# Attention with fp32 products: probabilities and values weighed without splitting, the first 28 units' scores from keys and queries as loaded

## The chip, the cores and the metric

One NeuronCore of a Trainium2 chip. The time is the device time of one execution in microseconds (us); less is better. The kernel of before was timed in three executions and profiled in a further one.

## What is computed

Attention with a window and sinks, then two feed-forward layers, all in fp32 (shapes: 2 batches, 8 heads, 768 positions, 64 wide; 4 sinks, window 128; 1536 tokens, model 512 wide, hidden 2048).

```python
scores = (1/8) * q @ k.T                      # per batch and head
keep = (key < n_sink) | (0 <= query - key < window)
a = softmax(where(keep, scores, -1e9)); attn = a @ v
x = relu(attn @ w_in)**2 @ w_out              # layer 1
h = x @ w2_in                                 # layer 2
g = (a0 + a1 h + a2 h^2 + a3 h^3) / (1 + |b0||h| + |b1|h^2)
out = g @ w2_out
```

## The kernel before

TensorE's fast type here, fp32r, holds only the high bits of an fp32 number. So every operand is split into a high part (written as fp32r) and a low part (the number minus the high part), and a product is three matmuls: high by high, high by low, low by high (`PASSES`). For the scores the key sits in rows 0 to 63 as high part and in rows 64 to 127 as low part, and the query stands twice, so two matmuls do (`bq_hi`, `bq_lo`, line 1169).

Attention is cut into 96 units `u`, each one head of one tile of 128 queries; 8 heads make a tile, 6 tiles a batch; i = (u // 8) % 6 is the tile's place in its batch. A unit looks at up to 288 keys: 32 sink columns, the 128 keys before, the 128 of its own place. Tiles with i = 0 look at 128 keys, with i = 1 at 256, the others at 288. Four units make a group `k`; keys, queries and values arrive by group. A unit goes through this chain, where slot `s` starts unit s and works on earlier ones:

- PE `score` (L1170), DVE `scores` (L920: scale, mask, minimum per row; it writes `bprobs`, in which a unit's columns are 4 elements apart), ACT `exp` (L649, in place)
- PE `turn_p` two slots later (L1185, and L1187 for the sinks of four units at once), ACT `pT_part` (L642: high part), DVE `pT_part` (L929: low part)
- PE `weigh` three slots later: for each tile of 128 keys three matmuls of 64 columns (L1202); each fourth unit with i of 2 or more adds three of 256 columns for the sinks (L1212). In all 176 key tiles and 16 sink products.
- per tile of queries: DVE `finish`, then `tile_out` (four transposes, a high part, a low part) into `xT`.

The first 28 units (`LEAD`) run alone, slot after slot. The other 68 are laid between the matmuls of layer 1 (`first1` L1125, `second1` L1137), at places given by `events` and `slot_of`, in blocks 0 to 2 of four. Layer 2 follows and touches no attention.

The splitting is done by several engines. POOL splits each group's keys and queries (`split_kq`: L439, L441, L443, L452), its values (`split_v`: L461, L464) and the sinks; for the first three groups ACT and DVE split the queries (`early_q`: L625, L828). The 16 weight tiles of layer 1 are split by ACT (high, L634) and POOL (low, L426), the low parts of the first two by DVE during the lead (L858). All DMAs are issued by SP in one order written out by hand (`banded`); `load_kq` and `load_v` wait until the split of two groups before has freed the buffer. Every engine enters `banded` through a branch on `path_ready`, which DVE sets at line 823.

## Time and profile before

| | us |
|---|---|
| median of three executions | 725.2 (723.95 to 727.53) |
| profiled execution | 728.82 |
| its span, first to last instruction | 726.8 |
| PE busy | 695.8 (96%) |
| DVE busy | 487.5 (67%) |
| ACT busy | 413.5 (57%) |
| POOL busy | 372.4 (51%) |

The profiled execution lies 2.0 us above its span and 3.6 us above the median. A timeline gives the start of an instruction, its time and its engine; several alike in a row are merged (x6), so the start of the next row tells how long they took in truth. A matmul's own time is modelled and includes the way through the array; for its price the distance of the starts is read. Most of the span falls to four stretches: the lead up to 67, blocks 0 to 2 of layer 1 with the other units up to 375, block 3 without units up to 443, then layer 2.

### The profile page before, as it was taken

Reading aid. Unit: us, or ns where it says so; the run is one execution under the profiler, and the core shown is the slowest. Engines: PE = TensorE matmul, PEld = TensorE weight load, DVE = VectorE, ACT = ScalarE, POOL = GpSimd, SP = SyncE. Lnnn points to the kernel's source line nnn. Section 1 sums busy time; section 2 is a strip of 40 time slices with the busy share of each in tenths; the row PEclk is TensorE's granted clock in tenths of the full one; section 3 lists DMA queues with packets and bytes.
Section 4 is the critical chain, followed back from the end, with each engine's and each line's share of the span. In section 5 each row is a group of like instructions: output and inputs, shape, how many; then the busy total and the mean of one; then the engine's idle time right before and its main releaser. Section 6 shows DMA issues by size and latency. Waiting matters only on the chain.

```text
span 726.8 us, 10617 instructions
## 1 busy us (share of the span) xinstructions
PE 695.8 (96%) x3888; PEld 662.6 (91%) x3888; DVE 487.5 (67%) x714; ACT 413.5 (57%) x861; POOL 372.4 (51%) x376
## 2 busy tenths in 40 slices
PE   3999989999999999999999997999999999999996
PEld 2998989999999999999999997889988998998995
DVE  6664465564465554554445665799989889898985
ACT  3764446554545544554432223677787787778774
POOL 5666157675242350530002221777867767776773
PEclk9999999999999999999999998999999999999999
DMA  6654211112221113100003332000210120001001
GB/s 204 212 216 158 86 37 37 44 37 73 88 88 37 37 37 124 37 8 1 1 1 130 131 116 92 1 1 1 88 43 1 45 86 1 1 1 43 1 1 44
DMA packets 14507, 43.50 MB, mean 60 GB/s; under 512 B 1648, under 2 KB 4976, under 8 KB 13936
## 3 DMA queue, kind: packets, MB, share of 16 engines
q1 hardware_dynamic: 14448, 42.74, 16.9%
q8 instruction: 34, 0.56, 0.3%
q14 instruction: 25, 0.20, 0.1%
HBM read 36.44 MB, written 6.29 MB: 59 GB/s over the span
## 4 chain that ended last, share of the span: by engine, by line
PE 84%; DVE 6%; POOL 4%; issue 3%; ACT 2%; DMA 1%; POOLq 0%; DVEq 0%; SPq 0%; ACTq 0%
PE h_ps L1125 22%; PE y_ps L1137 17%; PE y_ps L1356 16%; PE s_ps L1125 8%; PE o_ps L1202 6%; PE o_ps L1125 4%; PE s_ps L1170 3%; PE s_ps L1185 3%; PE y_ps L1202 1%; DVE s_ps L874 1%; DVE sq L837 1%; PE o_ps L1212 1%; PE y_ps L1170 1%; POOL weights L426 1%; DVE o_ps L874 1%
## 5 line engine op out<-in xcount | busy, mean ns | idle before, releaser
L1125 PE MATMUL h_ps<-xT,weights 128*128 128x384 f32 x960 | 194.8, 346 | 3.4 <-DVE xT L961 1.5
L1125 PEld LDWEIGHTS h_ps<-xT,weights 128*128 128x128 f32 x960 | 171.5, 192 | 6.2 <-issue 3.0
L1137 PE MATMUL y_ps<-hid,weights 128*128 128x384 f32 x768 | 156.3, 343 | 0.0
L1356 PE MATMUL y_ps<-weights,hid 128*128 128x512 f32 x576 | 144.7, 395 | 4.1 <-POOL hid L553 4.1
L1137 PEld LDWEIGHTS y_ps<-hid,weights 128*128 128x128 f32 x768 | 134.9, 190 | 0.0
L1356 PEld LDWEIGHTS y_ps<-weights,hid 128*128 128x128 f32 x576 | 107.1, 188 | 26.1 <-POOL hid L553 5.9
L649 ACT ACTIVATE bprobs<-bprobs,neg_max 128x288 f32<-128x288 f32 (+2 forms) x96 | 73.5, 766 | 58.4 <-DVE neg_max L920 56.9
L837 DVE TENSOR_TENSOR sq<-sq 128x384 f32<-128x384 f32 x64 | 44.6, 696 | 80.2 <-ACT sq L581 80.1
L439 POOL TENSOR_SCALAR bq_hi<-kq_raw 128x512 fp32r<-128x512 f32 x21 | 13.4, 640 | 148.0 <-PE s_ps L1170 132.2
L544 POOL TENSOR_TENSOR q_buf<-h_abs,q_buf 128x384 f32<-128x384 f32 x64 | 65.0, 1016 | 45.3 <-ACT q_buf L604 43.5
L553 POOL TENSOR_TENSOR hid<-p_buf,hid 128x384 fp32r<-128x384 f32 x64 | 65.6, 1025 | 41.2 <-ACT hid L760 40.8
L874 DVE RECIPROCAL s_ps<-q_buf 128x384 f32<-128x384 f32 x32 | 82.0, 2561 | 3.3
L843 DVE TENSOR_TENSOR hid<-sq,hid 128x384 fp32r<-128x384 f32 x64 | 55.8, 872 | 37.8 <-ACT hid L586 37.8
L581 ACT ACTIVATE sq<-h_ps 128x384 f32<-128x384 f32 x64 | 31.4, 491 | 79.8 <-PE h_ps L1125 79.7
L920 DVE CUSTOM_DVE_ANT_0 bprobs<-s_ps,band_bias 128x288 f32<-128x288 f32 (+2 forms) x82 | 51.2, 624 | 36.3 <-PE s_ps L1170 36.2
L1125 PE MATMUL s_ps<-xT,weights 128*128 128x384 f32 x384 | 73.7, 341 | 0.0
L1125 PEld LDWEIGHTS s_ps<-xT,weights 128*128 128x128 f32 x384 | 69.7, 191 | 2.6
L1202 PE MATMUL o_ps<-bv,bpT 128*128 128x64 f32 x456 | 70.5, 293 | 0.2 <-DVE o_sb L944 0.2
L548 POOL TENSOR_TENSOR p_buf<-p_buf,h_sb 128x384 f32<-128x384 f32 x64 | 65.0, 1016 | 0.0
L1202 PEld LDWEIGHTS o_ps<-bv,bpT 128*128 128x128 f32 x456 | 64.7, 212 | 0.3 <-issue 0.3
L421 POOL TENSOR_SCALAR weights<-weights_raw 128x1024 fp32r<-128x1024 f32 x16 | 16.8, 1052 | 90.0 <-DMA weights_raw<-in_w_pack 90.0
L586 ACT ACTIVATE hid<-sq 128x384 fp32r<-128x384 f32 x64 | 33.5, 524 | 48.8 <-DVE sq L837 48.8
(104 smaller groups left out, 1082.2 us busy)
## 6 DMA issues: line engine op xcount, KB each, us to landing
weights_raw<-in_w_pack SPq DMA_DIRECT2D x32, 512.0 KB, 3.7
kq_raw<-in_kq_pack SPq DMA_DIRECT2D x24, 512.0 KB, 3.9
bv_raw<-in_v_pack SPq DMA_DIRECT2D x24, 128.0 KB, 2.1
y_scratch<-xT SPq DMA_DIRECT2D x2, 1536.0 KB, 5.3
xT<-y_scratch SPq DMA_DIRECT2D x2, 1536.0 KB, 6.6
out_y<-out_stage SPq DMA_DIRECT2D x3, 768.0 KB, 3.5
out_y<-out_stage SPq DMA_DIRECT2D x3, 256.0 KB, 2.0
sink_raw<-in_vs_pack SPq DMA_DIRECT2D x2, 256.0 KB, 5.1
```

The costliest lines, as they stand in the source:

```text
L544: pool.tensor_tensor(q_buf[:, i % RING, :], h_abs[:, i % RING, :], q_buf[:, i % RING, :], ALU.mult).then_inc(qmul_ready, 1)
L548: pool.tensor_tensor(p_buf[:, i % RING, :], p_buf[:, i % RING, :], h_sb[:, i % RING, :], ALU.mult).then_inc(pmul_ready, 1)
L553: pool.tensor_tensor(hid2[:, i % RING, LO, :], p_buf[:, i % RING, :], hid2[:, i % RING, HI, :].bitcast(F32), ALU.subtract).then_inc(hid_re ...
L649: nc.scalar.activation(at, at, ACT.Exp, scale=-1.0, bias=neg_max[:, m:m + 1], accum_out=row_sum[:, qt % 2, m:m + 1]).then_inc(u_exp, 1)
L837: nc.vector.tensor_tensor(sq[:, i % 2, :], sq[:, i % 2, :], sq[:, i % 2, :], ALU.mult).then_inc(act1_ready, 1)
L843: nc.vector.tensor_tensor(hid[:, i % 2, LO, :], sq[:, i % 2, :], hid[:, i % 2, HI, :].bitcast(F32), ALU.subtract).then_inc(hid_ready, 1)
L874: nc.vector.reciprocal(h_banks[r], q_buf[:, r, :]).then_inc(qinv_ready, 1)
L920: nc.vector.tensor_tensor_reduce(out=bprobs[:, u // GROUP % 2, cols, m % GROUP], in0=score_bank(u)[:, cols], in1=band_bias[:, kind, cols], ...
L1125: ins = nc.tensor.matmul(bank, weights[:, i, wp, W_IN, t * P:(t + 1) * P], x, start=(t == 0 and n == 0), stop=(t == KC - 1 and n == 2))
L1137: ins = nc.tensor.matmul(y_ps[:, m, 0:NT], weights[:, i, wp, W_OUT, m * P:(m + 1) * P], hid[:, i % 2, gp, :], start=(i == 0 and n == 0), s ...
L1202: ins = nc.tensor.matmul(bank[:, D * m:D * (m + 1)], bpT[:, u % 2, pp, t * P:(t + 1) * P], bv[:, t, vp, D * m:D * (m + 1)], start=(m == 0 ...
L1356: ins = nc.tensor.matmul(y_bank(turn, t), hid2[:, i % RING, gp, t * P:(t + 1) * P], weights[:, i, wp, W_OUT, :], start=(i == 0 and n == 0) ...
```

## The change

- **Weighing.** `bpT` (three buffers instead of two) holds the turned probabilities whole in fp32, `bv` and `bvs` the values as loaded; a key tile is one fp32 matmul instead of three fp32r ones, a sink product too. One copy out of PSUM takes the place of high part and low part: by DVE for even units, by ACT for odd ones. `split_v` and `split_v_sinks` are gone, values are loaded straight into `bv`.
- **Scores of units 0 to 27.** One fp32 matmul of `q_raw3` with `bk_raw`, as loaded, instead of two on split operands; the lower half of these queries is zero. `early_q` and the splits of groups 0 to 6 are gone. From unit 28 on scores are as before, with `split_kq` on POOL; `split_earlier` makes up for the keys of groups 5 and 6 that units from 28 on still look at.
- **Score ring.** DVE writes the scaled scores to `bnegs`, four buffers with adjacent columns; `exp` reads them there and writes `bprobs`. The wait for the transposes of two groups before moves from DVE to ACT.
- **Weights of layer 1.** POOL does high and low part of the first four during the lead, ACT no high parts in it and DVE no low parts (`w_early` is gone). ACT does the high parts of weights 4 and 5 at the end of the lead, after a wait for POOL's four, then weight i + 6 in step i.
- **Loads.** Keys (128 x 4 x 128) and queries are separate DMAs, keys into four places of `bk_raw`. The order on SP is new; weights 2 to 4 come one at a time with groups 4 to 6, then two at a time, the last with group 12 (before: group 10).

```diff
-    EARLY_Q = 3
-    EARLY_W = 2
+    EARLY = LEAD // GROUP
+    EARLY_W = 4
+    P_RING = 3
+    N_RING = 4
...
-        bpT = sb("bpT", [P, 2, 2, 3 * P], F32R, band)
+        bpT = sb("bpT", [P, P_RING, 3 * P], F32, band)
...
             def load_v(k):
-                if k >= 2:
-                    sp.wait_ge(bv_ready, k - 1)
+                if 4 <= k:
+                    sp.wait_ge(u_pv, GROUP * (k - 1))
...
+            def load_k(k):
+                if EARLY + 2 <= k:
+                    sp.wait_ge(kq_ready, k - EARLY - 1)
+                elif 4 <= k:
+                    sp.wait_ge(u_scored, GROUP * (k - 1))
...
@@ POOL, banded @@
+                for i in range(2):
+                    weight_high(0, i)
+                    weight_low(i)
+                pool.wait_ge(ks_loaded, 16)
+                split_earlier(EARLY)
+                for i in range(2, EARLY_W):
+                    weight_high(0, i)
+                    weight_low(i)
+                split_earlier(EARLY + 1)
+                split_kq(EARLY)
+                split_kq(EARLY + 1)
...
@@ DVE @@
-                        out=bprobs[:, u // GROUP % 2, cols, m % GROUP], in0=score_bank(u)[:, cols],
+                        out=bnegs[:, u % N_RING, cols], in0=score_bank(u)[:, cols], in1=band_bias[:, kind, cols],
...
-                    dve.wait_ge(u_pT_high, u + 1)
-                    nc.vector.tensor_tensor(bpT[:, u % 2, LO, 0:cols], turn_bank(u)[:, 0:cols],
-                                            bpT[:, u % 2, HI, 0:cols].bitcast(F32), ALU.subtract
+                    dve.wait_ge(u_turned, u + 1)
+                    if u >= P_RING:
+                        dve.wait_ge(u_pv, u - P_RING + 1)
+                    nc.vector.tensor_copy(bpT[:, u % P_RING, 0:cols], turn_bank(u)[:, 0:cols]
...
@@ PE, score @@
+                    if k < EARLY:
+                        ins = nc.tensor.matmul(score_bank(u)[:, cols], q_raw3[:, k % 3, at], bk_raw[:, m, cols],
+                                               start=True, stop=True)
...
@@ PE, weigh @@
-                        for n, (pp, vp) in enumerate(PASSES):
-                            ins = nc.tensor.matmul(bank[:, D * m:D * (m + 1)], bpT[:, u % 2, pp, t * P:(t + 1) * P],
-                                                   bv[:, t, vp, D * m:D * (m + 1)],
+                        ins = nc.tensor.matmul(bank[:, D * m:D * (m + 1)], bpT[:, u % P_RING, t * P:(t + 1) * P],
+                                               bv[:, t, D * m:D * (m + 1)], start=(m == 0 and t == 0),
```

## Rows read from the trace of the kernel before

**Rows 1.** The page: the chain that ended last, by engine.

```profile
PE 84%; DVE 6%; POOL 4%; issue 3%; ACT 2%; DMA 1%; POOLq 0%; DVEq 0%; SPq 0%; ACTq 0%
```

**Rows 2.** Busy us (and instructions) of PE, PEld, DVE, ACT, POOL by stretch; PEclk, DMA.

```profile
26.00:67.00 41.00, 41.00 (x193) 40.92 (x191) 24.18 (x66) 25.84 (x60) 25.89 (x33) 1.00 0.58 210
...
187.00:282.00 95.00, 94.86 (x620) 94.41 (x619) 49.72 (x121) 46.83 (x111) 35.48 (x40) 1.00 0.18 62
```

**Rows 3.** Timeline of PE in the lead: start us, us, engine, line, what.

```profile
36.62 0.41 PE L1170 MATMUL y_ps<-bkT,bq_lo 128*128 128x256 f32 x1
36.83 0.63 PE L1185 MATMUL y_ps<-ident,bprobs 128*128 128x128 f32 x2
...
57.50 0.59 PE L1170 MATMUL s_ps<-bkT,bq_hi 128*128 128x288 f32 x1
57.89 0.44 PE L1170 MATMUL s_ps<-bkT,bq_lo 128*128 128x288 f32 x1
58.13 0.63 PE L1185 MATMUL s_ps<-ident,bprobs 128*128 128x128 f32 x2
58.41 1.47 PE L1202 MATMUL y_ps<-bv,bpT 128*128 128x64 f32 x6
59.69 0.59 PE L1170 MATMUL y_ps<-bkT,bq_hi 128*128 128x288 f32 x1
```

**Rows 4.** Timeline of PE in block 2, with layer 1 between the units.

```profile
310.24 0.83 PE L1202 MATMUL o_ps<-bv,bpT 128*128 128x64 f32 x6
310.91 1.30 PE L1137 MATMUL y_ps<-hid,weights 128*128 128x384 f32 x6
312.05 1.23 PE L1125 MATMUL h_ps<-xT,weights 128*128 128x384 f32 x6
313.12 0.30 PE L1170 MATMUL s_ps<-bkT,bq_hi 128*128 128x288 f32 x1
```

**Rows 5.** Timeline of PE from the end of the lead on.

```profile
69.72 4.18 PE L1125 MATMUL h_ps<-xT,weights 128*128 128x384 f32 x12 [1.50 <-DVE xT L961]
...
80.73 2.12 PE L1137 MATMUL y_ps<-hid,weights 128*128 128x384 f32 x6
82.66 0.33 PE L1170 MATMUL s_ps<-bkT,bq_hi 128*128 128x288 f32 x1
```

**Rows 6.** PE's largest group of weighing: busy us, mean ns of one, idle before.

```profile
L1202 PE MATMUL o_ps<-bv,bpT 128*128 128x64 f32 x456 | 70.5, 293 | 0.2 <-DVE o_sb L944 0.2
```

**Rows 7.** Timeline of all engines at the start.

```profile
5.20 0.15 DVE L823 CAST path<-in_band 128x1 int32<-128x1 f32 x1
...
7.15 0.89 DVE L895 TENSOR_SCALAR sq<-sq,limits 128x128 f32<-128x128 f32 x1 [0.32 <-issue]
...
9.03 0.62 POOL L441 TENSOR_SCALAR bkT<-kq_raw 128x512 fp32r<-128x512 f32 x1 [1.08 <-issue]
...
9.77 1.78 DVE L828 TENSOR_TENSOR bq_lo<-kq_raw,bq_hi 128x512 fp32r<-128x512 f32 x1
...
11.47 0.37 DVE L920 CUSTOM_DVE_ANT_0 bprobs<-s_ps,band_bias 128x128 f32<-128x128 f32 x1
```

**Rows 8.** Timeline of all engines at two gaps of PE in the lead.

```profile
18.57 0.85 PE L1202 MATMUL y_ps<-bv,bpT 128*128 128x64 f32 x3 [0.61 <-DVE bpT L929]
...
21.53 1.51 DVE L858 TENSOR_TENSOR weights<-weights_raw,weights 128x1024 fp32r<-128x1024 f32 x1
...
23.52 0.85 PE L1202 MATMUL y_ps<-bv,bpT 128*128 128x64 f32 x3 [0.68 <-DVE bpT L929]
```

**Rows 9.** Timeline of all engines in block 0, with PE's longest gap there.

```profile
81.50 0.56 DVE L837 TENSOR_TENSOR sq<-sq 128x384 f32<-128x384 f32 x1 [2.88 <-ACT sq L581]
...
95.76 5.03 POOL L426 TENSOR_TENSOR weights<-weights_raw,weights 128x1024 fp32r<-128x1024 f32 x2
...
95.93 2.62 DVE L837 TENSOR_TENSOR sq<-sq 128x384 f32<-128x384 f32 x1 [1.39 <-ACT sq L581]
...
101.84 0.40 PE L1170 MATMUL s_ps<-bkT,bq_hi 128*128 128x288 f32 x1 [2.04 <-DVE neg_max L920]
```

More of the change, by code:

```diff
@@ L190, in build @@
         w_high = sem("w_high")
-        w_early = sem("w_early")
         w_ready = sem("w_ready")
-        kq_loaded = [sem("kq_loaded0"), sem("kq_loaded1")]
-        bv_loaded = [sem("bv_loaded0"), sem("bv_loaded1")]
+        k_loaded = [sem(f"k_loaded{r}") for r in range(4)]
+        q_loaded = [sem("q_loaded0"), sem("q_loaded1"), sem("q_loaded2")]
+        bv_loaded = [sem(f"bv_loaded{r}") for r in range(4)]
         ks_loaded = sem("ks_loaded")
@@ L489, in _, with split_k @@
-            split_kq(0)
+            def split_k(heads, cols, done):
+                pool.tensor_scalar(bkT[:, heads, cols], bk_raw[:, heads, cols], 1.0, 0.0, ALU.mult, ALU.add
+                                   ).then_inc(bk_high, 1)
+                splits[0] += 1
+                pool.wait_ge(bk_high, splits[0])
+                pool.tensor_tensor(bkT[D:P, heads, cols], bk_raw[D:P, heads, cols],
+                                   bkT[D:P, heads, cols].bitcast(F32), ALU.subtract).then_inc(done, 1)
@@ new lines, in split_earlier, with split_sinks @@
+            def split_earlier(k):
+                pool.wait_ge(k_loaded[(k - 2) % 4], 16 * ((k - 2) // 4 + 1))
+                for cols in (own_cols(k - 2), slice(0, SINK_CAP)):
+                    split_k(heads_of(k), cols, bk_low)
+                    lows[0] += 1
+                    pool.wait_ge(bk_low, lows[0])
+            def split_sinks(bt):
+                pool.wait_ge(ks_loaded, 16 * (bt + 1))
+                pool.wait_ge(u_scored, H * KT * bt)
+                split_k(slice(0, H), slice(0, SINK_CAP), ks_ready)
+                pool.wait_ge(ks_ready, bt)
@@ L491, in banded @@
+            splits, lows = [0], [0]
             def banded():
-                pool.sem_inc(w_ready, EARLY_W)
                 def slot(s):
                     j, r = divmod(s, GROUP)
-                    if r == GROUP - 1:
-                        if j + 2 < GROUPS:
-                            split_kq(j + 2)
-                        if j + 1 < GROUPS:
-                            split_v(j + 1)
-                    if s == 7:
-                        split_k_sinks(0)
-                    if s == 11:
-                        split_v_sinks(0)
-                    if s == H * KT + 7:
-                        split_k_sinks(1)
-                    if s == H * KT + 11:
-                        split_v_sinks(1)
@@ L511, in banded @@
-                split_kq(1)
-                split_v(0)
-                for s in range(LEAD):
-                    slot(s)
-                weight_low(EARLY_W)
+                    if r == GROUP - 1 and j + 2 < GROUPS:
+                        split_kq(j + 2)
+                    if s == H * KT + 7:
+                        split_sinks(1)
+                for i in range(2):
[3 more added lines that the diff above has]
+                split_earlier(EARLY)
@@ L681, in banded @@
                         tile_out(s // H - 1)
-                    if s in (5, 13, 20, 24):
-                        weight_high((5, 13, 20, 24).index(s))
+                act.wait_ge(w_ready, EARLY_W)
+                for i in range(EARLY_W, EARLY_W + 2):
+                    weight_high(i)
                 relu(0, 0)
@@ L952, in slot @@
                         scores(s)
-                    if 2 <= s < U_ALL + 2:
+                    if 2 <= s < U_ALL + 2 and s % 2 == 0:
                         pT_part(s - 2)
@@ L1168, in score @@
                     cols = key_cols(i)
-                    for n, queries in enumerate((bq_hi, bq_lo)):
-                        ins = nc.tensor.matmul(score_bank(u)[:, cols], queries[:, r, at], bkT[:, m, cols],
-                                               start=(n == 0), stop=(n == 1))
+                    if k < EARLY:
+                        ins = nc.tensor.matmul(score_bank(u)[:, cols], q_raw3[:, k % 3, at], bk_raw[:, m, cols],
+                                               start=True, stop=True)
+                    else:
+                        for n, queries in enumerate((bq_hi, bq_lo)):
+                            ins = nc.tensor.matmul(score_bank(u)[:, cols], queries[:, k % 2, at], bkT[:, m, cols],
+                                                   start=(n == 0), stop=(n == 1))
                     ins.then_inc(u_scored, 1)
```

277 lines of the change are left out of this document (110 added, 167 removed).

## The prediction

> **What bounds the kernel now.** I read the page first: the chain that ended last is PE for 84% of the span [rows 1]. Then busy time by stretch, because a share over the whole span says nothing of a stage. In the lead, from 26 us on, PE is busy without a break, and in block 1 for 94.86 of 95 us, while DVE, ACT and POOL have half their time free or more [rows 2]. So work taken from those three pays only where PE waits for them, and what counts is the price of a product on PE. The reader is to see two more things in PE's timeline.
>
> Second, the clock. 12 products of 384 columns took about 3.84 us or 0.32 each after the lead, which is 384 columns at 1.2 GHz [rows 5]; in block 2 six took 1.07, 0.178 each, near 2.4 GHz [rows 4]. The granted clock column says 1.00 in both stretches [rows 2], but the distances say that the lead runs at the lower level. The higher level is there from about 82.66, where a product of 288 columns shows 0.33 instead of 0.59 [rows 3, 5]; the unbroken 3.84 us of products from 69.72 on did not bring it.
>
> **The unknown price.** The trace has no true fp32 product: the key tiles' products, three a tile, are fp32r, of which 456 stand in one group [rows 6], and so are the scores'. It must lie between one slot and four. One: four products of halves of 64 columns are 256 columns, which fit a slot. Four: each product of halves brings its own load. I take two: an fp32 weight has two halves, so two loads, and behind each of them the moving operand's halves pass, 2 x 64 columns, which the slot hides up to 256. Wider products cost 4 columns' time for each column: 1152 for 288. The two transposes of a unit, plain fp32 of 128 columns, get 0.43 together (unit of 2.19, less 0.48 for the score and 1.28 for the weighing) [rows 3], so reading fp32 weights needs no more than a slot. The Trainium skill, Perfetto Trace Analysis, Engine Utilization, halves TensorE's output rate for FP32_LOW_HIGH; with two passes that would be the two slots I take. No run here shows it yet.
>
> **Part by part**, against the profiled execution (728.8, span 726.8); the median of the timed ones is 3.6 lower.
>
> 1. *Weighing beside layer 1.* Of 176 key tiles 42 are weighed in the lead (units 0 to 24: 8x1 + 17x2), 134 later. Each goes from 3 slots to 2 at 0.112 [rows 4]: 134 x -0.112 = -15.0. PE is the bound there, nothing hides it or gives it back: DVE and ACT are half idle [rows 2]. 14 sink products of 256 columns go from 3 x 0.118 to 1024 columns at 0.178/384 each, 0.47: +0.12 x 14 = +1.7. Sum -13.3; bounds -29 (one slot), +17 (four).
> 2. *Lead, PE's work,* at 1.2 GHz. Units with i = 0 (8): score 2 slots before, 512 columns or 2 slots after; weighing 3 slots to 2: -0.213 each, -1.7. With i = 1 (8): score +2 slots (1024 columns), weighing two tiles -2 slots: 0. With i of 2 or 3 (12): score 2 x 0.24 to 1152 columns at 1.2 GHz, 0.96: +0.48, weighing -0.43: +0.05, +0.6. Two sink products: 0.64 to 0.85, +0.4. Sum -0.7.
> 3. *Start.* The first score's reading at 11.47 waited for masks from 7.15 and then for the query split at 9.77 (1.78) [rows 7]. Now there is no `early_q`; DVE passes the branch, which cost POOL 1.08, after 5.35 and begins masks near 6.4: reading near 9.1, -2.4. Bounds -3.5 (no neighbour slows the masks any more) and -0.7 (the keys' DMA, now with pieces of 512 bytes, lands late).
> 4. *Gaps in the lead.* The weight split by DVE (1.51) made PE wait until 23.52 [rows 8]: -1.1. A like gap ahead of 18.57 [rows 8] came from `early_q` of group 2: -1.0. But POOL now splits four whole weights in the lead. In block 0 such a split (2.5 each) and a DVE operation with both operands in SBUF stretched one another: the square took 2.62 where it took 0.56 before [rows 9]. Masks 1 to 3 are such operations. I take +1.5, from 0 to +4. Sum -0.6.
> 5. *Block 0.* The same clash cost PE 2.04 at 101.84 [rows 9]. POOL loses `split_v`, about 1.2 per group, and two of its 14 low parts, so some gaps go: -1, from -3 to +1. Weights come later in SP's order (the last with group 12), each at least one step of 6 us before it is used.
> 6. *No cost.* The score ring makes `exp` and L920 faster at best; both lie beside PE. The new wait of `exp` for the transposes of two groups before has behind it ACT's copies, which PE awaits, but those transposes were done four units ago. ACT's two high parts at the end of the lead (2.1) lie beside the 3.84 of `first1` [rows 5]; POOL, which it waits for, has some 14 us of work on the four weights (2.5 a low part [rows 9], a high part less) in the 58 of the lead. Without that cover relu would be 2 late. The new `split_kq` of group 7 comes after its keys land, two units before the lead ends, and before unit 28 stand a tile's transposes and 12 to 18 products of `first1`, 4 us and more [rows 5]; the loads of groups on SP wait for units already three or four slots behind.
>
> Sum: -13.3 - 0.7 - 2.4 - 0.6 - 1.0 = -18.0, so 710.8 for a profiled execution, and 725.2 - 18.0 = **707.2** for the median.
>
> **The rivals.**
>
> *Four slots for an fp32 tile (slower).* For: nothing in the rows excludes it, and the price of a slot here does not depend on columns. Then weighing beside layer 1 is 134 x +0.112 = +15.0, the sinks +1.7; the lead has i = 0: +0.43 +0.21, x8 = +5.1; i = 1: +0.43 +0.43, x8 = +6.9; i = 2, 3: +0.48 +0.43, x12 = +10.9; sinks +0.4. With -4.0 for start and gaps: +36, **761**. It decides from just over three slots on: at exactly three, item 1 is +1.7, the lead's scores +9.2, sinks +0.4, so +7.3 after the -4.0, **732**. That could come about if the loads of the two halves don't pass behind the products before them. Against: with loads hidden as now, two suffice. The Trainium skill, FP8 and Floating Point Precision, TensorE Precision Notes, gives true fp32 "4 passes through PE array"; read as four loads that is this rival, read as four streams it is also mine.
>
> *One slot.* -29 in item 1, and 42 tiles x -0.213 = -9 in the lead beside the rest: **684**. For: 256 columns fit. Against: two halves of weights in one load of the same length.
>
> *The clock rises in the lead.* The columns streamed per unit with i = 3 go from 2x288 + 2x128 + 6x64 = 1216 to 1152 + 256 + 4x64x2 = 1920, of 2.2 us, so PE is denser than before. If the higher level comes near 26 us, PE needs 1.1 per unit and the chain on ACT and DVE near 1.3; twenty units save 0.9 each, -18: **689**. Against: 3.84 us of unbroken products at 69.72 did not yet raise it [rows 5], and those are denser than the new lead.
>
> *It does nothing where it says.* If item 1 gives nothing and scores cost as much as they save, 722: little stands for that.
>
> **How the numbers follow.** Forecast 0.50; four slots 0.13, three 0.10, one slot 0.08, clock in the lead 0.16, nothing 0.03. The forecast's own range is 700 to 714 (items 3 to 5 at their ends). The range that holds 8 in 10 reaches down to one slot and the clock, 684, and up to three slots, 732. A measurement of this kernel tells 0.5%, 3.6 us, from no change. Faster: forecast, one slot, clock: 0.74. Slower: 0.23, the two rivals of three and four slots. Same: 0.03.
>
> **What would show it.** In the timeline of a unit in block 2, the distance from the first L1202 product to what follows two tiles: 0.45 us for two slots a tile, 0.22 for one, 0.9 for four (0.67 before). In the lead the score of 288 columns: 0.96 at 1.2 GHz, 0.48 if the clock rose. First read of a score by DVE near 9.1. The share of stretched DVE operations in masks tells item 4. The prediction is wrong at its root if an fp32 tile takes three slots or more, or if in block 2 some other engine ends PE's waits.

## The result and the profile after

| | before | after |
|---|---|---|
| median of the timed executions, same chip | 724.6 (4) | 682.9 (4) |
| lowest to highest | 723.2 to 727.5 | 679.2 to 685.4 |
| profiled execution | 728.82 | 685.41 |
| its span | 726.8 | 683.6 |
| end of the lead (first product of layer 1) | 69.72 | 47.43 |
| PE busy | 695.8 | 654.5 |
| DVE busy | 487.5 | 451.3 |
| ACT busy | 413.5 | 383.2 |
| POOL busy | 372.4 | 329.7 |

The changed kernel is faster: 0.9415 of the time before, 95% interval 0.9357 to 0.9474. That is 41.7 us where 18.0 were forecast, and 1.1 us below the low end of the range.

The page of after. The chain that ended last is still PE's for the most part, as in [rows 1]:

```profile
PE 81%; DVE 8%; issue 4%; ACT 3%; POOL 2%; DMA 1%; DVEq 0%; POOLq 0%; SPq 0%; ACTq 0%
```

Busy us (and instructions) of PE, PEld, DVE, ACT, POOL by stretch in after, then PEclk, DMA share and GB/s, as in [rows 2]:

```profile
11.70:18.50 6.80, 4.75 (x31) 4.00 (x30) 5.72 (x20) 3.50 (x13) 4.46 (x3) 1.00 0.76 253
18.50:25.30 6.80, 5.14 (x21) 4.40 (x21) 5.11 (x10) 2.94 (x7) 2.40 (x2) 0.50 0.50 154
25.30:45.00 19.70, 19.00 (x130) 17.21 (x130) 11.33 (x43) 14.45 (x39) 12.30 (x13) 1.00 0.60 186
```

From 25.3 to its end at 47.43 the lead takes 22 us, where it took 44 from 26 on before. The granted clock falls once in the lead, to half, from 18.5 to 25.3, and is then full up to 677. As before, the column alone isn't enough (it reads 1.00 where no level has been noted yet, as it did for the lead in [rows 2]; before's first note of the clock is of 82.7); the distances decide. PE's timeline of a unit with i of 2 or more in the lead of after, as in [rows 3]:

```profile
30.79 0.70 PE L1143 MATMUL s_ps<-bk_raw,q_raw 128*128 128x288 f32 x2
31.33 0.39 PE L1162 MATMUL s_ps<-ident,bprobs 128*128 128x128 f32 x2
31.55 0.56 PE L1179 MATMUL o_ps<-bv,bpT 128*128 128x64 f32 x4
31.95 0.70 PE L1143 MATMUL y_ps<-bk_raw,q_raw 128*128 128x288 f32 x2
```

A unit takes 31.95 - 30.79 = 1.16 us where it took 2.19, so the lead is at the higher level. The score product stands as two matmuls with 0.54 between its start and the next, the two key tiles as four with 0.40. In block 2 of after, as in [rows 4]:

```profile
309.12 0.29 PE L1147 MATMUL s_ps<-bkT,bq_hi 128*128 128x288 f32 x1
...
309.39 0.39 PE L1162 MATMUL s_ps<-ident,bprobs 128*128 128x128 f32 x2
309.62 0.56 PE L1179 MATMUL o_ps<-bv,bpT 128*128 128x64 f32 x4
310.01 0.65 PE L1186 MATMUL o_ps<-bvs,bpT 128*128 128x256 f32 x2
310.31 1.41 PE L1105 MATMUL y_ps<-hid,weights 128*128 128x384 f32 x6
311.56 0.68 PE L1093 MATMUL h_ps<-xT,weights 128*128 128x384 f32 x3
```

The weighing took 0.39 here where [rows 4] have 0.67. The end of the lead and the way to block 0, as in [rows 5]:

```profile
47.43 2.33 PE L1093 MATMUL h_ps<-xT,weights 128*128 128x384 f32 x12 [1.77 <-DVE xT L936]
50.42 1.30 PE L1093 MATMUL h_ps<-xT,weights 128*128 128x384 f32 x6 [0.67 <-ACT sq L570]
51.56 0.29 PE L1147 MATMUL s_ps<-bkT,bq_hi 128*128 128x288 f32 x1
...
53.55 1.22 PE L1105 MATMUL y_ps<-hid,weights 128*128 128x384 f32 x6
```

The groups that answer to [rows 6]: the weighing, by forms (busy us, mean ns of one | idle before).

```profile
L1179 PE MATMUL o_ps<-bv,bpT 128*128 128x64 f32 x304 | 43.5, 264 | 0.0
...
L1179 PE MATMUL y_ps<-bv,bpT 128*128 128x64 f32 x48 | 8.0, 277 | 2.3 <-DVE bpT L905 2.3
```

304 + 48 = 352 = 2 x 176: an fp32 matmul of the program is two matmuls on PE, each with a weight load of its own.

Where the 43.2 us between the two spans lie, from the first `first1`, the block starts (first `second1` of each), and the last `second1`:

| stretch | before | after | difference |
|---|---|---|---|
| start to the end of the lead | 69.7 | 47.4 | -22.3 |
| to block 0 | 11.0 | 6.1 | -4.9 |
| block 0 | 106.2 | 100.4 | -5.8 |
| blocks 1 and 2 | 191.6 | 184.4 | -7.2 |
| block 3 | 64.9 | 64.9 | 0 |
| layer 2 with its handover | 283.3 | 280.3 | -3.0 |

These are one profile of each. The second profile of before (e12 below) has 68.6, 8.2, 106.4, 191.6, 64.9 and 284.2, that of after (e14) 48.5, 6.1, 101.2, 183.1, 64.9 and 279.8: a stretch is good to about 1 us, the way to block 0 before only to about 3.

So 27 us came ahead of block 0, where 3.7 were expected, and 13 in blocks 0 to 2, where 14 were.

### The profile page after: what moved, and what is told of

It reads as the page before. It is cut to its first block, busy times and chain, and to the rows that moved or that the text cites. A ratio compares the mean times of both kernels' runs of the same rounds, so it can differ in the third digit from the quotient of the medians.

```text
span 683.6 us, 10143 instructions
## 1 busy us (share of the span) xinstructions
PE 654.5 (96%) x3696; PEld 616.4 (90%) x3696; DVE 451.3 (66%) x661; ACT 383.2 (56%) x806; POOL 329.7 (48%) x314
## 4 chain that ended last, share of the span: by engine, by line
PE 81%; DVE 8%; issue 4%; ACT 3%; POOL 2%; DMA 1%; DVEq 0%; POOLq 0%; SPq 0%; ACTq 0%
PE h_ps L1093 22%; PE y_ps L1105 17%; PE y_ps L1327 17%; PE s_ps L1093 8%; PE o_ps L1093 4%; PE o_ps L1179 4%; PE s_ps L1162 2%; PE s_ps L1147 2%; DVE sq L812 2%; DVE s_ps L849 1%; DMA y_scratch<-xT 1%; PE o_ps L1186 1%; PE s_ps L1143 1%; DVE o_ps L849 1%; DVE bnegs L895 1%
## 5 line engine op out<-in xcount | busy, mean ns | idle before, releaser
L1093 PE MATMUL h_ps<-xT,weights 128*128 128x384 f32 x960 | 190.5, 340 | 2.4 <-DVE xT L936 1.8
L1093 PEld LDWEIGHTS h_ps<-xT,weights 128*128 128x128 f32 x960 | 167.4, 188 | 4.6 <-issue 2.9
L1327 PE MATMUL y_ps<-weights,hid 128*128 128x512 f32 x576 | 146.4, 399 | 5.2 <-POOL hid L542 5.1
L632 ACT ACTIVATE bprobs<-bnegs,neg_max 128x288 f32<-128x288 f32 (+2 forms) x96 | 72.6, 757 | 69.6 <-DVE neg_max L895 69.4
L812 DVE TENSOR_TENSOR sq<-sq 128x384 f32<-128x384 f32 x64 | 47.6, 744 | 89.8 <-ACT sq L570 89.8
L818 DVE TENSOR_TENSOR hid<-sq,hid 128x384 fp32r<-128x384 f32 x64 | 55.6, 868 | 37.8 <-ACT hid L575 37.8
L462 POOL TENSOR_SCALAR bq_hi<-q_raw 128x512 fp32r<-128x512 f32 x17 | 11.1, 650 | 140.9 <-DMA q_raw<-in_q_pack 140.8
L438 POOL TENSOR_SCALAR weights<-weights_raw 128x1024 fp32r<-128x1024 f32 x20 | 21.0, 1052 | 107.8 <-DMA weights_raw<-in_w_pack 107.7
L1093 PE MATMUL s_ps<-xT,weights 128*128 128x384 f32 x384 | 72.5, 337 | 0.0
L895 DVE CUSTOM_DVE_ANT_0 bnegs<-s_ps,band_bias 128x288 f32<-128x288 f32 (+2 forms) x82 | 34.8, 424 | 36.0 <-PE s_ps L1147 29.4
L742 ACT ACTIVATE hid<-p_buf 128x384 fp32r<-128x384 f32 x64 | 33.6, 525 | 30.5 <-DVE p_buf L852 30.5
L593 ACT ACTIVATE q_buf<-h_abs,abs_b 128x384 f32<-128x384 f32 x64 | 45.4, 709 | 2.1
```

Source lines behind the costliest of these rows:

```text
L593: nc.scalar.activation(q_buf[:, i % RING, :], h_abs[:, i % RING, :], ACT.Identity, scale=abs_b[:, 1:2], bias=abs_b[:, 0:1]).then_inc(lin_r ...
L632: nc.scalar.activation(bprobs[:, u // GROUP % 2, cols, m % GROUP], bnegs[:, u % N_RING, cols], ACT.Exp, scale=-1.0, bias=neg_max[:, m:m + ...
L812: nc.vector.tensor_tensor(sq[:, i % 2, :], sq[:, i % 2, :], sq[:, i % 2, :], ALU.mult).then_inc(act1_ready, 1)
L818: nc.vector.tensor_tensor(hid[:, i % 2, LO, :], sq[:, i % 2, :], hid[:, i % 2, HI, :].bitcast(F32), ALU.subtract).then_inc(hid_ready, 1)
L895: nc.vector.tensor_tensor_reduce(out=bnegs[:, u % N_RING, cols], in0=score_bank(u)[:, cols], in1=band_bias[:, kind, cols], scale=-SCALE, s ...
L1093: ins = nc.tensor.matmul(bank, weights[:, i, wp, W_IN, t * P:(t + 1) * P], x, start=(t == 0 and n == 0), stop=(t == KC - 1 and n == 2))
```

## The experiments

The first question was why the clock rose. Three theories: A, the fp32 score products make the lead's stream dense enough; B, nothing about products does it, the lead's gaps were the reason (a product stream without `early_q` and DVE's weight splits is unbroken); C, the fp32 weighing does it. Most kernels below take fp32r stand-ins (`bq_hi`, `bq_lo`, `v_st`, written once by POOL). They cost something themselves: PE's first product of the kernel then waits until 8.2 instead of 6.22, as the waits of e3_both show (us in total, times, longest):

```profile
PE s_ps L1154 <- POOL v_st L504: 8.2, 1, 8.2
```

### Each product type by itself

e1_weigh3: three fp32r products in place of each fp32 one in the weighing, everywhere; scores of the lead stay fp32.

```diff
-        bpT = sb("bpT", [P, P_RING, 3 * P], F32, band)
+        bpT = sb("bpT", [P, P_RING, 3 * P], F32R, band)
...
-                        ins = nc.tensor.matmul(bank[:, D * m:D * (m + 1)], bpT[:, u % P_RING, t * P:(t + 1) * P],
-                                               bv[:, t, D * m:D * (m + 1)], start=(m == 0 and t == 0),
...
+                        for n in range(3):
+                            ins = nc.tensor.matmul(bank[:, D * m:D * (m + 1)], bpT[:, u % P_RING, t * P:(t + 1) * P],
+                                                   v_st[:, D * (m % 2):D * (m % 2 + 1)],
...
```

> The changed kernel, but every key tile and sink product is weighed with three fp32r products again, on stand-in values (a rounded copy of the first values), so its output is not the attention: the low parts are left out. Lead scores stay fp32. Item 1 of the prediction says: beside layer 1 134 x +0.112 less 14 x 0.12 = +13.3; in the lead 42 x +0.112 = +4.7 if its clock stays high. Theory A (the dense fp32 scores bring the high clock in the lead): 701, with the products of the lead still at 0.112 per slot from about 25 us on. Theory B (the clock rises because PE no longer waits for splits, whatever the type): the same 701. Theory C (the fp32 weighing brings the clock): the lead runs at 0.213 per slot, about +18 more, 719.

e2_score2: two fp32r products in place of each fp32 score product of the lead; weighing stays fp32.

```diff
-                        ins = nc.tensor.matmul(score_bank(u)[:, cols], q_raw3[:, k % 3, at], bk_raw[:, m, cols],
-                                               start=True, stop=True)
+                        for n in range(2):
+                            ins = nc.tensor.matmul(score_bank(u)[:, cols], bq_hi[:, 0, at], bq_lo[:, 0, cols],
+                                                   start=True, stop=True)
```

> The changed kernel, but each score of the first 28 units is two fp32r products on stand-in operands (rounded copies of the first queries), so its output is not the attention; weighing stays fp32. Theory A: the lead falls back to the lower clock, slots of 0.213; with 8 x 1.07 + 8 x 1.71 + 12 x 1.76 = 43 us of PE in it instead of the 39 that it took, total about 687. Theories B and C: the high clock comes all the same, and with 28 cheaper scores (0.27 instead of 0.54 for 288 columns) the lead is at most as long, total 677 to 683.

e3_both: both edits, so all products are fp32r in numbers as before, on the loads, splits and ring of after.

> Both edits at once: PE's products as in the kernel before, with the changed kernel's loads, splits and copies; stand-in operands, so the output is not the attention. Theories A and C (the fp32 products bring the clock): the lead at 0.213 per slot, 8 x 1.28 + 8 x 2.13 + 12 x 2.19 = 54 us and some 8 for sinks, tiles and gaps, ending near 68 instead of 47: +20, and +13 beside layer 1: 716. Theory B (shorter chains and no waits bring it): the lead at 0.112 per slot and near 40 us, total near 700.

Measured, with 723.6 for before on this chip: e2_score2 685.1 (684.4 to 686.4), ratio 0.9453 [0.9403, 0.9503]. e3_both 715.8 (714.7 to 718.5), ratio 0.9869 [0.9818, 0.9920]. e1_weigh3 gave 724.8, 726.2, 727.1 and once 701.2. Its four executions are not noise around one time: two levels of the same program lie some 25 us apart, so no single ratio is given for it. Its profile is of one of the longer executions, 726.2: there the lead ends at 72.5 and the clock rose only at 77.0. Of the execution with 701.2 there is no profile; that its clock rose in the lead is inferred from its time, which is what the expectation has for a lead at the higher level.

PE's timeline in the lead of e3_both: start us, us.

```profile
51.73 0.83 PE L1154 MATMUL s_ps<-bq_lo,bq_hi 128*128 128x288 f32 x2
...
52.63 1.47 PE L1191 MATMUL y_ps<-v_st,bpT 128*128 128x64 f32 x6
53.91 0.83 PE L1154 MATMUL y_ps<-bq_lo,bq_hi 128*128 128x288 f32 x2
```

2.18 a unit, as before: the low level, though PE has no break here. B falls. A falls as well, since e2_score2 has none of the fp32 scores and its profile has the full clock from 28.8 to 49.3 and a lead that ends at 48.0; its four executions lie within 2 us, so the others are taken to be alike. (Theory A's 687 for e2 is near the measured 685.1, so the total alone would not have told them apart; it is the profile that does.) C in its strict form would fall if e1_weigh3's one execution that was 25 us shorter, without any fp32 weighing, had risen. e3_both also prices what has nothing to do with the clock: its lead ends at 63.9, 5.8 before that of before (4.7 before that of e12), at the same level and in spite of the later start that the stand-ins cause.

### Can PE be filled up in the kernel before

e4_before_fill: the kernel before, with idle fp32 products of the identity (into `h_ps`, overwritten later) in front and in the first slots: 14, then 8, 1, 1, 3, 2, 1, 1 in slots 2 to 8 (nine in slots 3 to 8, where the expectation says ten).

```diff
+            def filler(n):
+                for _ in range(n):
+                    nc.tensor.matmul(h_ps[:, 0:P], ident[:, :], ident[:, :], start=True, stop=True)
+
+            filler(14)
...
                 for s in range(LEAD):
+                    filler({2: 8, 3: 1, 4: 1, 5: 3, 6: 2, 7: 1, 8: 1}.get(s, 0))
                     slot(s)
```

> The kernel before, with fp32 products of the identity put on PE where it waits: 14 at the start, 8 ahead of slot 2, 10 more ahead of slots 3 to 8. They compute nothing that is used. If the clock of the lead is only a matter of getting it up once (a level that holds under the lead's own 1216 columns per unit), it stays high from about 10 us on, slots of 0.112, the lead is then set by the chain on ACT and DVE near 1.4 per unit, and the total falls by 15 to 20 to about 707. If the fp32r lead is too thin to hold it, the slots fall back to 0.213 within some us and the total is 722 to 728.

720.3 (718.9 to 724.4), ratio 0.9957 [0.9926, 0.9988]. PE's timeline:

```profile
14.23 0.31 PE L1176 MATMUL s_ps<-bkT,bq_hi 128*128 128x128 f32 x1
14.37 0.27 PE L1176 MATMUL s_ps<-bkT,bq_lo 128*128 128x128 f32 x1
...
17.66 0.83 PE L1208 MATMUL y_ps<-bv,bpT 128*128 128x64 f32 x3
18.30 1.20 PE L1120 MATMUL h_ps<-ident 128*128 128x128 f32 x4
```

At 14.23 the two score products start 0.14 apart, at 17.66 three short ones take 0.64, 0.213 each. So the clock did rise (full from 8.2), fell at 15, and with this kernel's own stream did not come back before 73. To raise it is not enough; the stream behind it must hold it. The 3.3 us that the median gained, below the 722 that was expected at least, are not the lead's, which ends at 69.6 against 69.7. Layer 2 takes 279.4 instead of 283.3 here, as the gap at its start is absent (see the handover to layer 2 below), and block 0 takes 103.7 instead of 106.2.

### Where the fp32 weighing counts

e8_weigh3_main and e9_weigh3_lead split the first edit by place.

```diff
+                        if u >= LEAD - 3:      # e8; e9 has u < LEAD - 3
+                            for n in range(3):
+                                ins = nc.tensor.matmul(bank[:, D * m:D * (m + 1)],
...
+                        else:
+                            ins = nc.tensor.matmul(bank[:, D * m:D * (m + 1)],
+                                                   bpT[:, u % P_RING, t * P:(t + 1) * P].bitcast(F32),
```

> The changed kernel with three fp32r products per key tile and sink product only from unit 25 on, that is beside layer 1; stand-in values, so the output is not the attention. The lead keeps its fp32 weighing. Item 1 as predicted: +13.3, 696. If the gain was partly given back in gaps, as e1 against the changed kernel shows between the first product of block 0 and that of block 3 (294.1 against 284.7), then +9.4: 692. The lead's clock stays as in the changed kernel either way.

> The changed kernel with three fp32r products per key tile only in units 0 to 24, the lead; stand-in values, so the output is not the attention. Theory C (the fp32 weighing holds the lead at the higher level): the lead runs at 0.213 per slot most of the way and ends near 72 instead of 47, total near 708, with an execution now and then near 690 as e1 had one at 701. Without an effect on the clock only 42 x 0.112 = 4.7 are lost: 688.

e8_weigh3_main: 697.0 (695.0 to 698.7), ratio 0.9626 [0.9582, 0.9671] (before: 722.5 on this chip), with the lead ending at 47.9 as in after. Three slots instead of two cost 697.0 - 682.9 = 14.1, where item 1 has 13.3; after wasn't timed beside e8; e5_pool_later (below), which was, is 15.6 shorter. Its timeline in block 2:

```profile
305.25 0.39 PE L1172 MATMUL s_ps<-ident,bprobs 128*128 128x128 f32 x2
305.39 0.83 PE L1191 MATMUL o_ps<-v_st,bpT 128*128 128x64 f32 x6
306.06 0.60 PE L1208 MATMUL o_ps<-v_st,bpT 128*128 128x256 f32 x3
306.50 1.21 PE L1103 MATMUL h_ps<-xT,weights 128*128 128x384 f32 x6
```

From the transposes to behind the weighing 0.81, in after 309.39 to 310.01, 0.62: 0.19 for two tiles, close to two slots of 0.112 (0.22).

e9_weigh3_lead gave 710.5, 707.0, 686.1, 685.0: again two levels of one program, 23 us apart. Its profile is of 710.5, the lead at the low level to its end at 72.7; the shorter executions have no profile here either. The start of a unit there is

```profile
61.18 1.31 PE L1153 MATMUL y_ps<-bk_raw,q_raw 128*128 128x288 f32 x2
62.28 0.64 PE L1172 MATMUL y_ps<-ident,bprobs 128*128 128x128 f32 x2
```

The fp32 score takes 1.10 at the low level (0.96 was forecast for it) and 0.54 at the high one. So with fp32r weighing in the lead the rise sometimes comes and sometimes doesn't, as far as the times tell. Seven kernels have fp32 weighing there (after, e2, e5, e7, e8, e10, e13). The clock rose in the profile of each, and in those of e14 and e15, and no execution of any lies apart from the others by a step of this size.

### Is it the type or the stream

e11_dense_fp32r: e3_both with six fp32r score products per unit of the lead instead of two. No fp32 weighing or score at all, and more work for PE than e3_both.

```diff
-                        for n in range(2):
+                        for n in range(6):
                             ins = nc.tensor.matmul(score_bank(u)[:, cols], bq_hi[:, 0, at], bq_lo[:, 0, cols],
```

> e3, whose lead has no fp32 product and stayed at the low level, with six fp32r products per lead score instead of two, all on stand-in operands; the output is not the attention. Four more products per unit are pure extra work. If the high clock needs fp32 products, the lead stays low and takes 25 us more than in e3: about 741. If it is the stream of products without waits for weight loads, whatever their type, the level rises and the lead ends near 48 instead of 64: about 700, faster than e3 with more work.

709.4 (708.6 to 709.8), ratio 0.9791 [0.9759, 0.9823]: 6.4 below e3_both. That was on another chip (before: 724.1 there, 723.6 for e3_both) and the two ratio intervals just meet at 0.982, but the executions lie well apart: 708.6 to 709.8 against 714.7 to 718.5. PE's timeline of a unit:

```profile
50.79 1.04 PE L1154 MATMUL s_ps<-bq_lo,bq_hi 128*128 128x288 f32 x6
...
51.81 0.83 PE L1191 MATMUL y_ps<-v_st,bpT 128*128 128x64 f32 x6
52.48 1.04 PE L1154 MATMUL y_ps<-bq_lo,bq_hi 128*128 128x288 f32 x6
```

Four products more, and the unit takes 1.69 instead of 2.18: the high level, full from 26.0. The number type isn't needed: e11 has no fp32 work in the lead that e3_both hasn't too (the transposes), and the four added products alone brought the level. Only part of the gain over e3_both is the lead's, though: its lead ends at 60.2 against 63.9 (-3.7), and layer 2 begins without a gap that e3_both has (below). The 48 that was expected for the end of the lead left out that four more products of 288 columns cost 0.5 us per unit at the high level too.

What makes one stream dense enough and another not is open. It isn't the number of products: a unit of the lead that looks at 288 keys has 10 matmuls on PE in e3_both, which stays low, and 8 in e2_score2, which rises. Nor is it the columns per unit as the prediction's rival counts them: 1344 in e2_score2, which rises, and 1792 in e1_weigh3 and e9_weigh3_lead, which have it in one of four and two of four executions by their times. Why those two differ between executions isn't shown either.

### What POOL's weight splits in the lead cost

In after, two of them meet DVE (timeline of all engines):

```profile
13.73 2.41 POOL L443 TENSOR_TENSOR weights<-weights_raw,weights 128x1024 fp32r<-128x1024 f32 x1
...
14.19 2.19 DVE L859 TENSOR_SCALAR band_bias<-sq 128x32 bf16<-128x32 f32 x2
...
17.10 0.43 PE L1179 MATMUL y_ps<-bv,bpT 128*128 128x64 f32 x2 [1.82 <-DVE bpT L905]
...
18.63 2.36 POOL L443 TENSOR_TENSOR weights<-weights_raw,weights 128x1024 fp32r<-128x1024 f32 x1
18.75 2.26 DVE L911 TENSOR_SCALAR row_den<-row_sum 128x8 f32<-128x8 f32 x1
...
22.03 1.11 PE L1205 MATMUL y_ps<-ident,o_sb 128*128 128x128 f32 x4 [1.66 <-DVE o_sb L919]
```

The first of the two mask operations at 14.19 takes 1.99 of the 2.19 (for 32 columns), the one of `finish` on 8 columns 2.26, each beside a split, and PE stands for 1.82 and 1.66; at 18.5, between the two, the clock fell. That the first gap brought the fall fits the order but isn't tested by itself. The edits that move the splits:

```diff
+                pool.wait_ge(u_negs, 9)        # e5, e7: ahead of the first split
+            filler(10)                         # e7, e13: idle products at PE's start
+                pool.wait_ge(o_read, 1)        # e13, instead: ahead of weights 0 and 1
+                pool.wait_ge(o_read, 2)        # e13: ahead of split_earlier(EARLY)
```

Expected of e5_pool_later, which holds the splits back behind the masks:

> The changed kernel, but POOL starts on the weights only when DVE has read score 8, behind its masks. If the clash of item 4 (a mask operation of 0.2 that took 2.19 while POOL made a low part, PE waiting 2.2) is what costs, and the clock falls at 18.5 because of that gap, then -4 to -7: 676 to 679. If the clash only moves to finish and tile_out (each with DVE operations of the same kind): 682, no change.

Of e7_later_fill, e5 with idle products on PE at the start:

> e5 and ten fp32 products of the identity on PE before its first score, which compute nothing that is used. The clock should be up before the first units: they ran at 0.213 per slot up to 11.7. If PE sets the pace there, -1 to -2 against e5; if masks and the chain on DVE and ACT do, nothing against e5, and PE's fillers are free as it waits until 6.2 for the queries anyway.

Of e13_pool_around, with the idle products and the splits behind the first two tiles:

> The changed kernel with ten idle products at the start as in e7, and POOL's weights only after the first tile is finished by DVE, the splits for group 7 after the second. In e5 the clash had moved from the masks to the first finish (an operation of 0.16 took 1.70, PE waited 2.2). If POOL's low parts no longer meet either, -1 to -3 against e7: 676 to 678. If POOL is then late with the four weights, layer 1 starts late: over 683.

e5_pool_later 681.5 (679.2 to 683.0), 0.9410 [0.9365, 0.9455]: no difference to 0.9415 can be told. The masks are free, but the split now meets the `finish` of the first tile:

```profile
16.48 1.70 DVE L912 TENSOR_SCALAR row_den<-row_sum 128x8 f32<-128x8 f32 x1
```

The tile's transposes start only at 19.20, after PE stood for 1.93, so the second expectation came true: the clash moved.

e7_later_fill 678.9 (678.7 to 681.1), 0.9384 [0.9343, 0.9426], full clock from 5.1 on but for 18.8 to 22.2. e13_pool_around 679.2 (678.5 to 680.0), 0.9379 [0.9348, 0.9411]. Against after in its own run none of these intervals is clear, so after and the last of them were run on one chip with more executions, as e14_after_again and e15_pool_around_again:

> The changed kernel, unchanged, on the chip on which e13's twin runs. If its lead reaches the high level in every execution, all times lie within 678 to 687; if it sits at the edge as e9 did, one or more lie near 705. In its profile the lead ends between 44 and 51, no gap of 3.8 us at the change to layer 2.

> e13 again beside the changed kernel, on the same chip. Its lead ended at 41.7 instead of 47.4 and blocks 0 to 3 took 347.0 instead of 349.7; if that is its own and not the chip's, it is 3 to 5 us faster here too, about 679 against 683. If it was chance, both medians lie within 1.5 us.

e14_after_again 682.4 (680.7 to 685.4, six), 0.9405 [0.9378, 0.9432]; e15_pool_around_again 677.8 (676.9 to 682.8, six), 0.9360 [0.9328, 0.9392]. The intervals overlap a little, the medians are 4.6 apart and five of six executions of e15 lie below the lowest of e14. The lead of e15 ends at 41.6 against 48.5, and the same operation is

```profile
15.65 0.16 DVE L913 TENSOR_SCALAR row_den<-row_sum 128x8 f32<-128x8 f32 x1
```

0.16 instead of 2.26, and the clock of e15 is full from 7.2 through the whole lead. How much of the 4.6 is the idle products is open: e7 has them and e5 doesn't, on one chip, and e7 is 2.6 shorter with overlapping intervals. The version of e13 and e15 has the lowest median of all.

### The score ring

e10_no_ring: DVE writes `bprobs` with its columns 4 apart again and `exp` runs in place, the waits as before.

```diff
-                        out=bnegs[:, u % N_RING, cols], in0=score_bank(u)[:, cols], in1=band_bias[:, kind, cols],
+                        out=bprobs[:, u // GROUP % 2, cols, m % GROUP], in0=score_bank(u)[:, cols], in1=band_bias[:, kind, cols],
```

> The changed kernel without the score ring: DVE writes the scores into the strided probability buffer and exp works there in place, as before. The prediction costed the ring at nothing. Now that the lead runs at the high level, one unit takes about 1.16 us there and a score's reading on DVE 0.46 instead of 0.68: if the chain on DVE and ACT sets the lead's pace, 28 x 0.2 at most comes back, +2 to +5: 685 to 688. If PE sets it, 683.

687.2 (680.0 to 688.8), 0.9460 [0.9395, 0.9525] against 0.9415 [0.9357, 0.9474]: the intervals overlap, and one of its four executions is as fast as after. Its profile has the clock at half from 23.4 to 30.2 and from 50.7 to 54.1. The expectation's 685 to 688 holds it, but after's own executions reach 685.4: the ring may be worth some us by way of gaps in the lead; that isn't settled.

### The kernel before once more

> The kernel before, unchanged, profiled a second time. If the lead's low level and the gap of 3.8 us at the change to layer 2 (ahead of an o_ps product at 449) are the program's own, both stand again, first layer product near 70 and the gap near 445. If they are chance, one of them is missing.

725.9. The lead is low again (full only from 73.5) and ends at 68.6; the gap at the start of layer 2 is there again, 3.50 us ahead of 445.42. So neither is chance of one execution.

## Why the prediction was wrong, and where it was right

**What bounds the kernel, and the two readings of it.** Right. Slots price short matmuls, at 0.213 and 0.112, and the lead ran at the lower level, in both profiles of before.

**The unknown price.** Right, two slots. The counts show two matmuls and two weight loads for one fp32 product (352 for 176 tiles), and four of 64 columns take 0.39 or 0.40. So the rivals of one, three and four slots fell together. For 288 columns the score took 0.54 at the high level; forecast 0.48. That is 0.27 for each of its two matmuls, where the fp32r products of 288 columns at 309.12 take 0.135 each. The Trainium skill, Perfetto Trace Analysis, Engine Utilization, halves TensorE's output rate for FP32_LOW_HIGH, which agrees with that if it is taken for each of the two matmuls. The Trainium skill, FP8 and Floating Point Precision, TensorE Precision Notes, has "4 passes through PE array" for true fp32: read as four loads that doesn't agree with the counts, read as four streams it agrees with the 0.54, four times 0.135.

**Item 1, weighing beside layer 1, -13.3.** Right in its price, and near in its sum: 14.1 by e8_weigh3_main as a whole. But that agreement is in part luck. Between lead and block 0 e8 lost 3.0 (9.1 against 6.1), with the clock at half from 48.8 to 55.6. That isn't the weighing's: e2_score2 and e5_pool_later, whose layer 1 is that of after, have such a stretch too (49.3 to 56.1, 46.2 to 53.0) and take 8.9 there. In blocks 0 to 2 e8 lost 9.6 (294.4 against 284.8). The trace has 132 of the 134 tiles in these blocks, so the slots would be 132 x 0.112 - 1.7 = 13.1. Of the 3.5 that are missing 3.0 are idle time of PE, 5.8 in after against 2.8 in e8. Over all profiles these blocks take 293.4 to 294.4 in the four with three slots and the splits of after (e1, e3, e8, e11) and 280.9 to 284.8 in the nine with two slots. Two of the gaps in after that e8 doesn't have:

```profile
81.81 5.35 POOL L443 TENSOR_TENSOR weights<-weights_raw,weights 128x1024 fp32r<-128x1024 f32 x2
...
82.86 2.07 DVE L818 TENSOR_TENSOR hid<-sq,hid 128x384 fp32r<-128x384 f32 x1 [0.59 <-ACT hid L575]
...
85.36 0.40 PE L1147 MATMUL s_ps<-bkT,bq_hi 128*128 128x288 f32 x1 [1.23 <-DVE neg_max L895]
...
178.95 0.48 PE L1162 MATMUL s_ps<-ident,bprobs 128*128 128x128 f32 x2 [1.08 <-DVE xT L936]
```

"Nothing gives it back" was thus not quite true: a faster PE runs into DVE here and there.

**Item 2, the lead's work on PE, and the rival of the clock.** This is the step that failed. The item took 1.2 GHz for given; for that level its prices were near (1.10 for a score instead of 0.96), and so the lead that was to lose 0.7 there lost far more. The rival was on the table, with a denser stream on PE as its mechanism and a unit of 1.1 to 1.3 (measured 1.16), at a chance of 0.16. What spoke against it was wrong: that 3.84 us of unbroken products at 69.72 had not raised the clock, so a lead less dense would not either. Those 3.84 us came behind a break of 1.5 us, and the full level did come at 82.7, 13 us after their start; in e12, the same kernel, it came at 73.5, 4.9 us after the same first product. The row said nothing of a longer stream. In place of the step, e3_both (low) against e2_score2 (high) and e11_dense_fp32r (high without fp32 scores or weighing in the lead) show that what PE is given per unit decides whether the level rises; new loads and splits alone didn't raise it. The rival's own count, columns per unit, doesn't order the runs, so it was right in the main and not in its measure. The size: against e3_both, the same loads and splits at the low level, the lead of after is 16.5 shorter (47.4 against 63.9), of which 2.0 are the stand-ins' later start, so 14.5; the rival has 18. Beside this the item's own sum counts the weighing of units 25 to 27 in the lead as well as in item 1; with the 18 tiles of units 16 to 24 it would be +0.6 instead of -0.7.

The rival's total, 689 for a measured 682.9, lacks what follows the lead, because it priced the lead's units only. The clock also gives back what is at the low level before on the way to block 0: 11.0 became 6.1 (-4.9), products of 384 columns going from 0.32 to 0.19 each. This size holds for this pair of profiles; in e12 the way took 8.2.

**Item 3, start, -2.4.** Measured -3.8, the first reading at 7.63 instead of 11.47, just beyond the bound of -3.5.

```profile
4.81 0.15 DVE L805 CAST path<-in_band 128x1 int32<-128x1 f32 x1
...
6.00 0.29 DVE L870 TENSOR_SCALAR sq<-sq,limits 128x128 f32<-128x128 f32 x1 [1.03 <-issue]
...
6.22 0.77 PE L1143 MATMUL s_ps<-bk_raw,q_raw 128*128 128x128 f32 x2 [6.22 <-DMA q_raw<-in_q_pack]
...
7.63 0.29 DVE L895 CUSTOM_DVE_ANT_0 bnegs<-s_ps,band_bias 128x128 f32<-128x128 f32 x1
```

Masks begin at 6.00 instead of 7.15, and the first takes 0.29 where 0.89 stood in [rows 7]. The branch cost about what was taken from POOL's row (1.03). `path_ready` itself came 0.4 earlier, which was not foreseen.

**Item 4, gaps in the lead, -0.6.** The clash was foreseen at +1.5 (0 to +4). It showed in masks and also, not foreseen, in `finish`, 1.82 and 1.66 of idle PE. Avoiding it gives 4.6 (e15 against e14), idle products at the start and a clock that doesn't fall included, so it was nearer to the upper bound. The lead of e3_both says that items 3 and 4 together are -4.7 to -5.8 at the low level, in spite of the stand-ins (forecast -3.0).

**Item 5, block 0, -1.** Too small. Block 0 lost 5.8. By the slots its 46 tiles and 6 sink products are -4.4 of it, which would leave -1.4. But the kernels with three slots and the splits of after (e1, e3, e8, e11) take 101.4 to 102.5 there, so what isn't weighing is -3.7 to -4.8, beyond the bound of -3, and the weighing brought less than its slots in this block, where PE idles for 4.3 us in after. Part of it is that the clock before was at half from 103.2 to 106.6 behind the gap of [rows 9]; e4, the kernel before without such a stretch, takes 103.7 for the block.

**Item 6, no cost.** Nothing to the contrary was seen. DVE gains more than was thought, and PE doesn't see it in blocks 1 and 2.

**Not in the prediction: the handover to layer 2, -3.0.** The last products of layer 1 and the first of layer 2, PE's timeline, in before:

```profile
445.00 0.62 PE L1125 MATMUL o_ps<-xT,weights 128*128 128x384 f32 x2 [1.17 <-issue]
449.08 2.40 PE L1125 MATMUL o_ps<-xT,weights 128*128 128x384 f32 x7 [3.46 <-issue]
```

and in after:

```profile
405.02 2.35 PE L1093 MATMUL o_ps<-xT,weights 128*128 128x384 f32 x12 [1.40 <-issue]
```

PE waited 3.46 for nothing that the profile shows, and then the clock was at half for a while (447.9 to 454.8). This idle time is in before, e12, e1_weigh3 and e3_both (3.55 at 438.91 there) and in none of the others. e11_dense_fp32r differs from e3_both, and e4_before_fill from before, by PE instructions of the start and the lead alone, and they don't have it, so it isn't a matter of layer 1 or its data. The four that have it are those with 3888 matmuls on PE. In each of the four traces one packet of the instruction queue falls into the idle time:

```profile
q8 instruction: 1, 0.02, 1.9%
```

(before, 445.6 to 449.1: packets, MB, share of 16 engines); it starts at 446.77, takes 1.04, and PE goes on 1.3 us behind its end. No such packet starts within a gap of PE at this place in the other twelve. That PE waited there for its instructions is my guess from this; no run takes it apart.

**The chances.** The range missed by 1.1 us at its low end, which was the lower of two rivals each alone. The rival of the clock has to be summed with everything that changes level with it; with the way to block 0 as measured it gives 689 - 4.9 = 684. The last 3.0, the handover, nothing in the rows foretold. The rival of three slots leaves out 1.7 for the scores of the eight units with i = 0: 734 instead of 732.

## What to carry to other kernels

Read a stretch's clock level from distances, and price a change at both levels if it changes how dense PE's stream is: here that was worth more than the matmuls that were saved, and adding products to the fp32r stream made its lead 3.7 us shorter. When a rival is a change of level, sum it over every stretch up to the point where the level was high before, and ask what evidence a short stretch really gives. With PE made faster, look for POOL operations over SBUF beside small DVE operations on the critical chain; moving them by a wait on a step of DVE is cheap. And compare stretches, not totals: e4 and e11 owe much of their gain to the absence of a gap at the start of layer 2, which their edits weren't about.

## What the runs showed of the hardware

- Two levels of time of one program on one core, 23 to 25 us apart (e1_weigh3, e9_weigh3_lead). In the profiles of the longer ones the lead is at the low level to its end; that the clock rose in the shorter ones is inferred.
- PE and its weight loads can be busy without a break at the low level: 33.6 and 33.3 of 34 us in e3_both from 26 on; and idle products that raise the clock (full from 8.2 in e4) don't keep it up when the stream behind them is thin (half from 15.0 to 73.0).
- An fp32 matmul of 64 or 128 columns is two loads and two matmuls, and takes two slots of 0.1 to 0.11 at the high level (e13's ten idle products of 128 columns are 20 matmuls, 0.11 apart from 5.0 on); of 288 columns 0.54, and 1.10 at the low level.
- DVE operations on 8 to 32 columns in SBUF took 1.7 to 2.3 us beside a POOL operation on 1024 columns, 0.16 alone (row_den in e15). Beside two POOL operations of 5.35 us together from 81.81 on, DVE's reading of scores out of PSUM at 84.85 took 0.45, as everywhere.
- DVE's reading of scores of 288 columns with its minimum: 453 ns with adjacent output columns where it was 675 with columns 4 apart (675 again in e10_no_ring); `exp` on ACT 816 and 824 ns, no difference.

```profile
L895 DVE CUSTOM_DVE_ANT_0 bnegs<-s_ps,band_bias 128x288 f32<-128x288 f32 x58 | 26.3, 453 | 26.7 <-PE s_ps L1147 22.9 <-PE s_ps L1143 3.8
```
